# Attention scores' maxima in eleven pieces of up to 512 columns, and an earlier turn of the finished output

## The reference, cut to what matters

```python
q_pool = q.reshape(B, H, S // 2, 2, D).mean(axis=3)          # 576 queries a head
scores = scale * np.matmul(q_pool, k.transpose(0, 1, 3, 2))  # 576 x 1152
scores = scores - np.max(scores, axis=-1, keepdims=True)
attn = np.exp(scores)
attn = attn / (np.sum(attn, axis=-1, keepdims=True) + 1e-09)
return np.matmul(attn, v)
```

## Time and profile before

| | |
|---|---|
| median of three runs | 1187.63 us |
| profiled execution | 1186.41 us |
| its span, first to last instruction | 1184.6 us |
| attention stage (32 heads) | about 0 to 530 us |
| granted TensorE clock, mean | 0.99 of 2.4 GHz |
| TensorE / VectorE / ScalarE / GpSimd busy | 95% / 68% / 52% / 57% |

### The profile page before, as it was taken

One profiled execution on the slowest core, in us unless ns is written; L12 is line 12 of the kernel. 1 busy time (PEld: TensorE's weight loads), 2 busy tenths in 40 slices (PEclk: granted clock), 3 DMA queues, 4 the chain that ended last, 5 costly groups with the idle time before them and its releaser, 6 DMA issues. The chain is left out here.

```text
span 1184.6 us, 19899 instructions
## 1 busy us (share of the span) xinstructions
PE 1122.5 (95%) x7088; PEld 930.8 (79%) x7088; DVE 806.1 (68%) x1574; ACT 620.6 (52%) x1228; POOL 673.6 (57%) x687
## 2 busy tenths in 40 slices
PE   6999999989999999998898989789999999999998
PEld 5877777777788777787777777568888898888987
DVE  5888877767888888866556565665448754686554
ACT  4666665566666666655565656632334333443331
POOL 5888899998888888744332335503334333633330
PEclk9999999999999999998999999999999999999999
DMA  8221111211112121001001011123221522223121
GB/s 206 61 61 57 48 53 58 60 43 50 61 61 61 60 61 41 22 1 36 2 1 41 2 38 62 54 87 95 71 72 54 169 64 71 71 64 114 54 71 54
DMA packets 76593, 71.47 MB, mean 60 GB/s; under 512 B 11856, under 2 KB 54864, under 8 KB 76496
## 3 DMA queue, kind: packets, MB, share of 16 engines
q1 hardware_dynamic: 75888, 69.90, 19.7%
q10 hardware_dynamic: 608, 0.30, 0.1%
HBM read 60.74 MB, written 9.44 MB: 59 GB/s over the span
## 5 line engine op out<-in xcount | busy, mean ns | idle before, releaser
L647 DVE TENSOR_REDUCE part_max<-psA 128x1 f32<-128x384 f32 x465 | 250.5, 556 | 60.8 <-PE psA L382 38.0
L576 ACT ACTIVATE pT<-psA 128x576 f32<-128x576 f32 x288 | 187.8, 652 | 164.4 <-PE psA L401 155.1
L270 POOL TENSOR_TENSOR pT<-pT 128x576 f32<-128x576 f32 x157 | 225.3, 1435 | 24.8 <-ACT pT L576 2.8
L382 PE MATMUL psA<-kT,qT 128*128 128x384 f32 x465 | 166.2, 379 | 9.8 <-DVE part_max L647 9.3
L2149 DVE TENSOR_TENSOR hidden_parts<-psC,hidden_parts 128x384 f32<-128x384 f32 x168 | 91.1, 554 | 122.3 <-PE psC L1999 114.9
L415 PE MATMUL psA<-pT,v_raw 128*64 128x288 f32 x1152 | 153.8, 412 | 0.0
L1826 POOL TENSOR_TENSOR w_raw<-w_raw 128x256 f32<-128x256 f32 x24 | 18.3, 762 | 232.3 <-DMA w_raw<-in_moe_w_ch 232.1
L392 PE MATMUL psA<-qT,kT 128*128 128x288 f32 x576 | 132.9, 312 | 0.0
L401 PE MATMUL psA<-qTm,kT 128*128 128x288 f32 x576 | 124.0, 297 | 0.5 <-ACT qTm L562 0.5
L415 PEld LDWEIGHTS psA<-pT,v_raw 128*64 128x64 f32 x1152 | 77.0, 136 | 53.2 <-issue 6.4
L392 PEld LDWEIGHTS psA<-qT,kT 128*128 128x128 f32 x576 | 99.0, 190 | 18.2 <-issue 14.0
(11 more groups left out here) (196 smaller groups left out, 2610.3 us busy)
## 6 DMA issues: line engine op xcount, KB each, us to landing
w_raw<-in_moe_w_ch SPq DMA_DIRECT2D x48, 256.0 KB, 3.1
k_raw<-in_k SPq DMA_DIRECT2D x32, 288.0 KB, 2.9
v_raw<-in_v SPq DMA_DIRECT2D x32, 288.0 KB, 2.8
q_raw<-in_q SPq DMA_DIRECT2D x31, 256.0 KB, 3.3
w_even<-in_moe_w_ch SPq DMA_DIRECT2D x12, 512.0 KB, 5.0
w_odd<-in_moe_w_ch SPq DMA_DIRECT2D x12, 512.0 KB, 4.9
u_rows<-x_all SPq DMA_DIRECT2D x16, 256.0 KB, 2.0
u_even<-u_rows SPq DMA_DIRECT2D x2, 1536.0 KB, 7.0
```

Of the source, the lines that this page charges most:

```text
L270: nc.gpsimd.tensor_tensor(pT[:, KT, :], pT[:, KT, :], pT[:, j, :], ALU.add).then_inc(part_summed, 1)
L382: nc.tensor.matmul(maxes[n % 2][:, 0:PIECE], qT[h % 3][:, t * P:(t + 1) * P], kT[u][:, c * PIECE:(c + 1) * PIECE], start=True, stop=True). ...
L576: nc.scalar.activation(pT[:, j, :].rearrange("p (a c) -> p a c", a=2), scores[n % 2][:, :, 0:HALF], ACT.Exp, scale=0.5 * float(D) ** -0.5) ...
L647: nc.vector.tensor_reduce(part_max[u][:, t, c:c + 1], maxes[n % 2][:, 0:PIECE], AX.X, ALU.max).then_inc(max_freed[n % 2], 1)
```

## The change

PIECES now has eleven entries. Four ("a", t) are the full query tiles t = 0 to 3 against keys 0 to 511, four ("b", t) the same against keys 512 to 1023. ("c", None) holds four matmuls of 128 columns, the tiles 0 to 3 against keys 1024 to 1151, side by side in one bank, with one reduction into four columns. The last query tile has 64 queries; `qT` gets a second copy of it (L546 writes 256 columns instead of 128), so that columns 512 to 639 are the queries and then zeros, and columns 576 to 703 are zeros and then the queries. ("half", 0) and ("half", 1) accumulate two matmuls each: the rows 0 to 63 then hold the queries against keys 0 to 575, the rows 64 to 127 the same queries against keys 576 to 1151; the first has 512 columns, the second 64. `maximum` waits for both banks, copies the two columns of the rows 64 to 127 to the rows 0 to 63 (a new VectorE copy of 64 x 2 elements), waits for that copy, and reduces four columns for each tile instead of three. `part_max` has four columns; those that are not written hold the lowest value, from two new memsets at the start.

TensorE's order within a head: the query turn moves in front of piece 3, score 3 in front of piece 4, score 4 in front of piece 5; the output's turn, the row sum and the early values follow piece 5; then pieces 6 and 7, score 5, piece 8, the "ka" turn, score 6, piece 9, score 7, piece 10, score 8. VectorE normalises in front of piece 6. In the last head the output's turn, row sum and normalising of head 30 move behind the turn of the fifth tile of x.

```diff
-    PIECES = ([(t, c) for c in range(2) for t in range(QT - 1)] + [(QT - 1, 0), (QT - 1, 1)]
-              + [(t, 2) for t in range(QT)])
+    PIECES = ([("a", t) for t in range(QT - 1)] + [("b", t) for t in range(QT - 1)]
+              + [("c", None), ("half", 0), ("half", 1)])
+    HALF_KEYS = S // 2
...
-        qT = [sb(f"qT{u}", [P, WIDE], F32R) for u in range(3)]
+        qT = [sb(f"qT{u}", [P, WIDE + P], F32R) for u in range(3)]
-        part_max = [sb(f"part_max{u}", [P, QT, 3]) for u in range(2)]
+        part_max = [sb(f"part_max{u}", [P, QT, 4]) for u in range(2)]
...
-                nc.tensor.matmul(maxes[n % 2][:, 0:PIECE], qT[h % 3][:, t * P:(t + 1) * P],
-                                 kT[u][:, c * PIECE:(c + 1) * PIECE], start=True, stop=True
-                                 ).then_inc(max_filled, 1)
+                if kind == "half":
+                    a, z = ((0, BANK), (BANK, HALF_KEYS))[t]
+
+                    parts = [(out[:, 0:z - a], q[:, c:c + P],
+                              k[:, m * HALF_KEYS + a:m * HALF_KEYS + z])
+                             for m, c in enumerate(((QT - 1) * P, SQ))]
+                elif kind == "c":
+                    parts = [(out[:, t * P:(t + 1) * P], q[:, t * P:(t + 1) * P], k[:, 2 * BANK:S])
+                             for t in range(QT - 1)]
+                else:
+                    at = 0 if kind == "a" else BANK
+                    parts = [(out, q[:, t * P:(t + 1) * P], k[:, at:at + BANK])]
+                for m, (to, queries, keys) in enumerate(parts):
+                    mm = nc.tensor.matmul(to, queries, keys, start=kind != "half" or m == 0,
+                                          stop=kind != "half" or m == 1)
+                mm.then_inc(max_filled, 1)
...
                 score(h, 2)
-                maxima(3, 4)
                 if more2:
                     turn_queries(h + 2)
+                maxima(3, 4)
+                score(h, 3)
                 maxima(4, 5)
-                score(h, 3)
+                score(h, 4)
                 maxima(5, 6)
+
                 if h > 0:
                     turn_out(h - 1)
-                maxima(6, 7)
-                if h > 0:
                     sum_rows(h - 1)
-                maxima(7, 8)
-                score(h, 4)
+                values(h, range(EARLY))
+                maxima(6, 8)
+                score(h, 5)
                 maxima(8, 9)
-                values(h, range(EARLY))
-                maxima(9, 11)
-                score(h, 5)
-                maxima(11, 12)
                 if more2:
                     turn_keys(h + 2, "ka", range(0, 4))
-                maxima(12, 13)
                 score(h, 6)
-                maxima(13, 14)
+                maxima(9, 10)
                 score(h, 7)
-                maxima(14, 15)
+                maxima(10, 11)
                 score(h, 8)
...
-                    nc.scalar.activation(qT[h % 3][:, 4 * P:WIDE], turn[:, P:2 * P], ACT.Copy)
+                    nc.scalar.activation(
+                        qT[h % 3][:, 4 * P:].rearrange("p (n c) -> p n c", c=P),
+                        turn[:, P:2 * P].unsqueeze(1).to_broadcast([P, 2, P]), ACT.Copy)
...
-                nc.vector.tensor_reduce(part_max[u][:, t, c:c + 1], maxes[n % 2][:, 0:PIECE],
-                                        AX.X, ALU.max).then_inc(max_freed[n % 2], 1)
+                if kind == "half":
+                    to = part_max[u][:, QT - 1, t:t + 1]
+                    src = src[:, 0:BANK if t == 0 else HALF_KEYS - BANK]
+                elif kind == "c":
+                    to = part_max[u][:, 0:QT - 1, 2]
+                    src = src.rearrange("p (t k) -> p t k", k=P)
+                else:
+                    c = 0 if kind == "a" else 1
+                    to = part_max[u][:, t, c:c + 1]
+                nc.vector.tensor_reduce(to, src, AX.X, ALU.max).then_inc(max_freed[n % 2], 1)
...
-                    dve.wait_ge(max_freed[n % 2], n // 2 + 1)
+                    for m in (n - 1, n):
+                        dve.wait_ge(max_freed[m % 2], m // 2 + 1)
+
+                    nc.vector.tensor_copy(part_max[u][0:LAST, QT - 1, 2:4],
+                                          part_max[u][LAST:P, QT - 1, 0:2]
+                                          ).then_inc(halves_moved, 1)
+                    dve.wait_ge(halves_moved, h)
...
+            nc.vector.memset(part_max[0][:, :, 3:4], LOWEST).then_inc(padded, 1)
+            nc.vector.memset(part_max[1][:, :, 2:4], LOWEST).then_inc(padded, 1)
...
-                    if at == 9 and h > 0:
+                    if at == 6 and h > 0:
                         normalise(h - 1)
```

More of the change, by code:

```diff
@@ L30 @@
 MASKED = -1000000000.0
+LOWEST = -3.0e38
 def ceil_div(a, b):
@@ L154, in attention @@
         wide_reduced = sem("wide_maxima_reduced")
+        halves_moved = sem("halves_moved")
         padded = sem("padding_written")
@@ L182, in attention @@
         block = ctx.enter_context(nc.Block())
-        PADS = 8
+        PADS = 10
         def load_q(eng, h):
@@ L372, in max_piece @@
             def max_piece(h, at):
-                u, (t, c) = h % 2, PIECES[at]
+                u, (kind, t) = h % 2, PIECES[at]
                 n = max_no(h, at)
+                out, q, k = maxes[n % 2], qT[h % 3], kT[u]
                 if at == 0:
                     pe.wait_ge(qa_copied, h + 1)
-                for first, name in (((0, 0), "ka"), ((0, 1), "kb"), ((QT - 1, 0), "kc")):
-                    if (t, c) == first:
+                for first, name in ((("a", 0), "ka"), (("b", 0), "kb"), (("c", None), "kc")):
+                    if PIECES[at] == first:
                         pe.wait_ge(turn_freed, keys_before[name, h] + 1)
@@ L499, in _ @@
             first(0, ("x", 2))
-            turn_out(h - 1)
-            sum_rows(h - 1)
             first(0, ("x", 3))
@@ L504, in _ @@
             first(0, ("x_last",))
+            turn_out(h - 1)
+            sum_rows(h - 1)
             values(h, range(EARLY))
@@ L644, in max_piece @@
             def max_piece(h, at):
-                u, (t, c), n = h % 2, PIECES[at], max_no(h, at)
+                u, (kind, t), n = h % 2, PIECES[at], max_no(h, at)
+                src = maxes[n % 2]
                 dve.wait_ge(max_filled, n + 1)
-                nc.vector.tensor_reduce(part_max[u][:, t, c:c + 1], maxes[n % 2][:, 0:PIECE],
-                                        AX.X, ALU.max).then_inc(max_freed[n % 2], 1)
+                if kind == "half":
[8 more added lines that the diff above has]
+                nc.vector.tensor_reduce(to, src, AX.X, ALU.max).then_inc(max_freed[n % 2], 1)
             def wide_maxima(t):
                 dve.wait_ge(wide_filled, t + 1)
-                nc.vector.tensor_reduce(part_max[0][:, t, :], wide(t), AX.X, ALU.max
+                nc.vector.tensor_reduce(part_max[0][:, t, 0:3], wide(t), AX.X, ALU.max
                                         ).then_inc(wide_reduced, 1)
@@ L760, in _ @@
             first(0, ("x", 2))
-            normalise(h - 1)
             first(0, ("x", 3))
             first(0, ("x_last",))
+            normalise(h - 1)
             add_tile(5, 0)
```

## The result

The changed kernel took 1216.23 us (median of four runs) against 1186.97 before in the same session: a ratio of 1.0237, 95% interval 1.0219 to 1.0255. The forecast was 1183.7; the first rival, with a chance of 0.17, had 1217.

What follows compares the result with a forecast made beforehand. TensorE was taken as busy 15.31 of a head's 15.33 us, with 1.6 us of stalls and exposed loads. A head falls from 15.32 to 15.15: 0.17 x 22 = 3.7, plus 0.2 for the first head, giving 1183.7 us; range 1172 to 1200.

Steps and rivals of the forecast that it cites:

- the first rival: The added copy misses GpSimd's pause and waits until 13.19; period 16.65, +29 us, 1217; chance 0.17.
- Which heads count: Attention stage: 22 heads can gain; seven long heads, held by GpSimd's splitting of expert weights, count for nothing.
- VectorE's pieces: Maxima in a head: ten of 0.69 us and one of 0.22 cost 7.12 instead of 8.34, 1.2 us less.
- Start and middle: Head's first score matmul (T=0) through the early values: values start at 5.36 instead of 5.75 and end at 7.45.
- Behind the values: From piece 6 to the last turn: stall of 0.18 at piece 8, score 6 until 9.90, last turn until 11.82.
- End of the maxima: Added copy issued at 11.55 in GpSimd's pause, done 11.72; maximum ends 11.93, TensorE resumes 12.03, period 15.13.
- my walk: Step-by-step timing of one plain head; some ten terms of about 0.1 us could each be absent or doubled: 15.0 to 15.3.
- The page that spoke against the change: Trace and skill: VectorE copies in two-port mode wait out GpSimd's whole instruction, reductions never; only the added copy is exposed.
- Rival 2: TensorE's exposed loads at pieces 2, 3, 8 and stall at 8 vanish: period about 14.9, 1178 us; chance 0.18.
- Once only: Start-up memsets, wider L546 and last head's moved turn, row sum and normalising: together nothing, within 0.3.
- Rival 3's loop: GpSimd's additions, L668, row sums, piece 0: if the key copy comes 0.3 later, period stays 15.3, 1187; chance 0.15.

Runs made afterwards that it cites:

- the version that beats both: Changed kernel with the small copy written as a reduction and the turn of the keys of h+2 in front of piece 8: 1182.47 us, ratio 0.9951.
- the kernel before with the spare copy: Kernel before plus a 64 x 2 copy into an otherwise unused tile and a wait for it in front of each final maximum: 1216.24 us, ratio 1.0239.

## Why the prediction was wrong

- *Which heads count.* Right: of 28.3 us between the first and last plain head, 0.6 lie in the seven long heads and the one after them. The seven alone take 119.7 us, as before.
- *VectorE's pieces.* Right: 214.6 us for 341 maxima; 0.69 us for 512 columns in every row.
- *Start and middle.* Right: values at T=5.36 and piece 6 at 7.45, as written, with two errors of 0.1 (turn and row sum) that cancelled.
- *Behind the values.* **Here the step failed by its size.** "0.26 of piece 8, the turn (0.27), an exposed load, score 6 until 9.90" was 0.47, 0.34 and 10.24. Piece 8 started 0.09 late and score 6 took 0.03 less than charged, which with the 0.21 and 0.07 makes 0.34 us. I had charged the four short matmuls of piece 8 at the pace of transposes, 0.065 each; they took 0.12 each, with the stall in front of them and, in the version that beats both, without.
- *End of the maxima.* "A copy issued at 11.55 falls into the pause" is the sentence that was wrong. It was issued at 11.89; piece 10 ended at 11.79 instead of 11.51, and the copy followed it by 0.10 instead of 0.04. The pause was at 11.64 to 11.78, where I had it (11.62 to 11.77). The kernel with the keys' turn in front of piece 8 issues it at 11.55 in the mean and is what I had described: 15.12 for a forecast of 15.15.
- *The mechanism.* Right, as rival 1: wait until 13.19 (13.18 measured), TensorE again at 13.55 (13.52), period 16.65 (16.62), 1217 (1216.23). What I got wrong was its chance. I held a margin of 0.15 us against "the errors of my walk", some ten terms of 0.1, and gave the miss 0.17. Ten independent errors of 0.1 spread by about 0.3 us, and an error beyond 0.15 on the late side then has a chance of about one in three; that is an estimate from my own terms. I also counted on heads erring apart. In nine plain heads the copy was issued between T=11.86 and 11.93, so that nearly all miss or nearly all hit, and the range should not have stopped at 1200.
- *The page that spoke against the change* held. L691 as a copy waits and as a reduction never does (31 of 31 at 0.15 us), as the Trainium skill, SBUF — State Buffer, section Who interferes with whom, has it. Of the two rows that I gave for it, L668 comes out by its own numbers (207.52 for 207.53); L724 ended 0.08 behind the memset, where 128 columns at my 1.05 ns would need 0.13.
- *Rival 2* (the stalls shrink more) did not happen: even without the copy the period is 15.38. *Once only* was "nothing, within 0.3"; the last head took 0.2 to 1.3 us more than before in the kernels with the changed order (18.65 us without the copy, 19.55 with it, 18.28 before).
- *Rival 3's loop* (GpSimd's additions, row sums, piece 0) was not what holds the period: with that chain 0.18 us earlier it stays at 15.1.
- *Slips in the sums.* The list of a head's matmuls adds up to 13.55 us, not 13.7, and the chances to 0.50 faster and 0.26 same, not 0.53 and 0.23. Neither changed the forecast.

## What to carry to other kernels

Before adding even a 64 x 2 copy from SBUF to SBUF on VectorE in front of a wait that TensorE hangs on, look at what GpSimd does at that moment: if a long GpSimd instruction runs there, price the copy at what is left of that instruction, or write it as a reduction over one element, which did not wait in any of the runs here. Where a schedule repeats exactly, a margin is a coin thrown once for all heads: set it against the spread of the whole walk, not against one term. And work that looks free to move (a turn, a row sum) may be free only because it stands in a wait.

## What the runs showed that I had not expected

A copy waits for a running GpSimd instruction even if it moves only two elements on 64 partitions, and though the two share no tile: in the kernel before with the spare copy it took 1.03 us in the head shown, beside 0.165 for a copy that met a pause in the changed kernel. A copy issued in the last 0.14 us of an addition, or in the 0.14 us pause behind it, is as fast as alone, and the addition behind it starts on time (351.44, 0.15 behind the one before, as elsewhere). Four matmuls of 128 columns took 0.47 us, where four transposes in a row go by in about 0.3.
